# Second MoE's up products by seven block products instead of eight, with x2 kept in fp32

## What is computed

```
logits = x2 @ w_gate;  P = exp(logits - logits.max())
for _ in range(8):
    P /= P.sum(1, keepdims=True) + 1e-09
    P /= P.sum(0, keepdims=True) + 1e-09
    P *= N / E
for e in range(E):
    h = np.maximum(x2 @ w1[e], 0.0)
    out += P[:, e:e + 1] * (h @ w2[e])
```

## Time and profile before

| | |
|---|---|
| median of 3 runs | 1305.37 us (1305.13 to 1306.25) |
| the profiled execution | 1304.42 us, of which 1302.6 us are the span |
| mean granted TensorE clock | 1.00 of full speed |
| PE busy | 1265.2 us, 97% of the span, 8109 matmuls |
| DVE, ACT, POOL busy | 50%, 35%, 28% |

### The profile page before, as it was taken

How to read it: one execution, slowest core, us unless ns; L and a number is a source line. 1 busy time by engine, 2 the same in 40 slices (tenths; PEclk the granted TensorE clock), 3 DMA queues, 4 the chain that set the end, 5 groups by cost and what they waited for, 6 DMA issues and landing times.

```text
span 1302.6 us, 21366 instructions
## 1 busy us (share of the span) xinstructions
PE 1265.2 (97%) x8109; PEld 1119.5 (86%) x8109; DVE 653.2 (50%) x1557; ACT 458.6 (35%) x960; POOL 365.7 (28%) x319
## 2 busy tenths in 40 slices
PE   6999999999999999999999999999999999999999
PEld 5777787887887998899899899898898898998997
DVE  5999999999998237322222222222222222222222
ACT  4776666766766233022022032031131130220210
POOL 2774434524434223033032031131131130230300
PEclk9999999999999999999999999999999999999999
DMA  4875664654544643021021120020120220210001
GB/s 129 275 245 181 255 221 127 231 186 171 208 178 156 259 162 98 1 65 50 17 65 33 32 64 32 32 64 17 48 64 1 64 64 0 64 60 5 0 0 72
DMA packets 72929, 130.14 MB, mean 100 GB/s; under 512 B 42016, under 2 KB 42016, under 8 KB 63648
## 3 DMA queue, kind: packets, MB, share of 16 engines
q1 hardware_dynamic: 72864, 129.27, 29.3%
HBM read 110.12 MB, written 19.14 MB: 99 GB/s over the span
## 4 chain that ended last, share of the span: by engine, by line
PE 79%; DVE 16%; ACT 1%; SPq 1%; DMA 1%; issue 1%; POOL 1%; ACTq 0%; DVEq 0%
PE banks L409 25%; PE banks L411 24%; PE banks L410 24%; DVE stats L862 7%; DVE rest L873 6%; PE banks L477 2%; PE banks L444 1%; PE banks L453 1%; DVE g_f L927 1%; PE banks L470 1%; DMA q_nat<-in_q_dram 1%; SPq L333 1%; PE banks L500 0%; ACT pT L705 0%; PE banks L425 0%
## 5 line engine op out<-in xcount | busy, mean ns | idle before, releaser
L822 ACT ACTIVATE h_hi<-banks 128x384 fp32r<-128x384 f32 x192 | 94.4, 492 | 624.7 <-PE banks L411 624.7
L409 PE MATMUL banks<-x_lo,wu_hi 128*128 128x384 f32 x768 | 257.2, 335 | 0.0
L411 PE MATMUL banks<-x_hi,wu_hi 128*128 128x384 f32 x768 | 256.8, 334 | 0.0
L410 PE MATMUL banks<-x_hi,wu_lo 128*128 128x384 f32 x768 | 256.8, 334 | 0.0
L988 DVE SCALAR_TENSOR_TENSOR h_lo<-banks,h_hi 128x384 fp32r<-128x384 f32 x192 | 106.8, 557 | 281.7 <-ACT h_hi L822 281.7
L1087 POOL TENSOR_TENSOR wu_lo<-wu_raw,wu_hi 128x512 fp32r<-128x512 f32 x76 | 95.9, 1299 | 526.1 <-ACT wu_hi L761 519.1
L1030 DVE SCALAR_TENSOR_TENSOR y_acc<-banks,plan_e,y_acc 128x512 f32<-128x512 f32 x135 | 101.3, 751 | 272.3 <-PE banks L411 272.3
L409 PE MATMUL banks<-wd_lo,h_hi 128*128 128x512 f32 x576 | 227.9, 396 | 0.0
L411 PE MATMUL banks<-wd_hi,h_hi 128*128 128x512 f32 x576 | 227.8, 396 | 0.0
L410 PE MATMUL banks<-wd_hi,h_lo 128*128 128x512 f32 x576 | 227.8, 396 | 0.0
L862 DVE MAX8 stats<-rest 128x8 f32<-128x576 f32 x216 | 156.1, 750 | 0.7
(11 more groups left out here) (103 smaller groups left out, 1804.7 us busy)
## 6 DMA issues: line engine op xcount, KB each, us to landing
wu_raw<-in_moe_w_dram SPq DMA_DIRECT2D x32, 512.0 KB, 3.7
wd_raw<-in_moe_w_dram SPq DMA_DIRECT2D x32, 512.0 KB, 3.7
wu_hi<-kept_up_hi SPq DMA_DIRECT2D x14, 1024.0 KB, 5.6
wu_lo<-kept_up_lo SPq DMA_DIRECT2D x14, 1024.0 KB, 8.0
wd_hi<-kept_down_hi SPq DMA_DIRECT2D x14, 1024.0 KB, 6.3
wd_lo<-kept_down_lo SPq DMA_DIRECT2D x14, 1024.0 KB, 8.4
q_nat<-in_q_dram SPq DMA_DIRECT2D x64, 72.0 KB, 2.3
wu_raw<-in_moe_w_in_dram SPq DMA_DIRECT2D x8, 512.0 KB, 5.3
```

What stands on the lines that cost most here:

```text
L409: pe.matmul(to, a_hi, b_lo, start=first, stop=False)
L410: pe.matmul(to, a_lo, b_hi, start=False, stop=False)
L411: return pe.matmul(to, a_hi, b_hi, start=False, stop=last)
L822: act.activation(h_hi[:, f, CH * c:CH * (c + 1)], ps_up[:, at % UBANKS, 0:CH], ACT.Relu).then_inc(h_hi_done, 1)
```

## The change

- **Up products.** The 2x2 blocks are: D in two halves (256 each), hidden columns in two halves (256 of a unit's 512), tokens in two halves (576 each). Strassen's scheme in Winograd's form makes the four output blocks from 7 products of block sums instead of 8 products. A unit is 4 cells; a cell is one of 2 blocks of 128 hidden columns by one of 2 token quarters of each half (288 tokens). A cell has 7 products of 6 matmuls with 288 columns: 168 matmuls for each unit.
- **Outputs.** Products 0 to 3 fill four banks, 4, 5 and 6 are added by PE onto banks 0, 2 and 3. ACT copies product 0 out (P1); DVE forms U2, U3, H22, H21, H12 in SBUF with five additions; ACT makes four ReLUs and DVE four low parts of 288 columns.
- **Weights.** w1 is summed on POOL (4 operations of 128x512 for each unit), cast in 7 pieces on ACT and lowered in 7 pieces on POOL, into one buffer instead of two; the casts wait for the unit's last up product. w2 keeps two slots; its four casts stand on ACT after cell 2.
- **x2.** It stays fp32, so `sums_high`, `sums_low` and `split_sums` go. Its 7 operands for each of 2 token quarters are summed on DVE (4), cast on ACT (7) and lowered on DVE (7), 128x576 each: for c = 0 in steps 85 to 90, for c = 1 two at step 98 to 100, the rest after x2 is complete.
- **Logits.** 36 fp32 matmuls with x2 as weights and 8 columns moving, after x2 is complete, write the transposed logits straight away. The two chunks at step 88 go.
- **Down products.** Tiles go in the order 0, 1, 5, 2, 3, 4, 6, 7, 8; the first three need only cells 0 and 1. `y_acc` shares its memory with x2. Units 0 and 1 are added unscaled, and 9 `scale_tile` operations of DVE scale the sum after unit 1. The plan's rounds: two `column_sums` in unit 0's up part, three in its down part, three in unit 1's up part.

```diff
+PRODUCTS = 7
+BANK_OF = (0, 1, 2, 3, 0, 2, 3)
+CELLS = [(f, c) for c in range(2) for f in range(2)]
+DOWN_TILES = (0, 1, 5, 2, 3, 4, 6, 7, 8)
+EARLY_TILES = 3
...
 # PE
+            def logits_of(t):
                 for a in range(KD):
+                    last = pe.matmul(ps_gate[:, E * t:E * (t + 1)], x2[:, a, P * t:P * (t + 1)], gate_raw[:, a, :],
+                                     start=a == 0, stop=a == KD - 1)
...
+            def product(he, cell, i):
+                f, c = CELLS[cell]
+                k = len(CELLS) * he + cell
+                if i == 0:
+                    need(pe, h_lo_done, 4 * (k - 1) + 2)
+                elif i == 1:
+                    need(pe, summed, 5 * (k - 1) + 1)
+                elif i == 2:
+                    need(pe, summed, 5 * (k - 1) + 4)
+                elif i == 3:
+                    need(pe, summed, 5 * k)
+                elif i == 4:
+                    pe.wait_ge(p1_copied, k + 1)
+                else:
+                    pe.wait_ge(summed, 5 * k + i - 3)
+                if cell == 0:
+                    pe.wait_ge(lo_split["up"], up_lows(UQ + he) + i + 1)
+                for a in range(2):
+                    last = three_passes(ps_up[:, BANK_OF[i], 0:QT], w1_hi[:, i, a, cols], w1_lo[:, i, a, cols],
+                                        xo_hi[c][:, i, a, :], xo_lo[c][:, i, a, :], i < 4 and a == 0, a == 1, i >= 4)
...
 # ACT
+            for place in range(2, PRODUCTS):
+                x_high(1, place)
+            act.wait_ge(xo_lo_done, 2 * PRODUCTS)
...
+            def cell_high(he, cell):
+                need(act, summed, 5 * (k - 1) + 1)
+                act.wait_ge(up2_done, PRODUCTS * k + 1)
+                act.copy(parts_f32[:, P1, :], ps_up[:, 0, 0:QT]).then_inc(p1_copied, 1)
+                act.wait_ge(summed, 5 * k + 3)
+                relu(2 + f, tokens_of(1, c), parts_f32[:, H22, :])
+                act.wait_ge(up2_done, PRODUCTS * k + 5)
+                relu(f, tokens_of(0, c), ps_up[:, 0, 0:QT])
+                act.wait_ge(summed, 5 * k + 4)
+                relu(2 + f, tokens_of(0, c), parts_f32[:, H21, :])
+                act.wait_ge(summed, 5 * k + 5)
+                relu(f, tokens_of(1, c), parts_f32[:, H12, :])
             def expert(he, slot, first, last):
+                for cell in range(len(CELLS)):
+                    cell_high(he, cell)
+                    if cell == 2 and not last:
...
+                        w2_high(he + 1, 1 - slot)
+                if not last:
+                    act.wait_ge(up2_done, PRODUCTS * len(CELLS) * (he + 1))
+                    for i in range(PRODUCTS):
+                        w1_high(he + 1, i)
...
 # DVE
+            def cell_sums(he, cell):
...
+                add(part[U2], bank[1], part[P1])
+                add(part[U3], bank[2], part[U2])
+                add(part[H22], bank[3], part[U3])
+                low(2 + f, tokens_of(1, c), part[H22])
+                low(f, tokens_of(0, c), bank[0])
+                add(part[H21], bank[2], part[U2])
+                add(part[H12], bank[3], part[U2])
+                low(2 + f, tokens_of(0, c), part[H21])
+                low(f, tokens_of(1, c), part[H12])
...
+            def scale_tile(at):
+                t = DOWN_TILES[at]
+                dve.wait_ge(y_added, TT + at + 1)
+                dve.tensor_scalar(y_acc[:, t, :], y_acc[:, t, :], plan[:, t, 0:1], None,
+                                  ALU.mult).then_inc(y_added, 1)
...
 # POOL
             with pool.Fori(1, E) as e:
                 for half in range(HALVES):
-                    split("up", UQ + HALVES * e + half, half)
-                    split("down", UQ + HALVES * e + half, half)
+                    w2_lows(HALVES * e + half, half)
+                    w1_sums(HALVES * e + half)
+                    w1_lows(HALVES * e + half)
```

More of the change, by code:

```diff
@@ L47 @@
 NU2 = E * HALVES
-CH = 384
-NCH = N // CH
 TT = N // P
 SLOTS = 2
-UBANKS, DBANKS = 4, 3
-ROUND_AFTER = [(3, 3), (5, 1), (6, 3), (8, 1), (9, 3), (11, 1)]
+DBANKS = 3
+PRODUCTS = 7
+BANK_OF = (0, 1, 2, 3, 0, 2, 3)
+HF = UNIT // 2
+CELLS = [(f, c) for c in range(2) for f in range(2)]
+DOWN_TILES = (0, 1, 5, 2, 3, 4, 6, 7, 8)
+EARLY_TILES = 3
+U2, U3, H22, H21, H12, P1 = range(6)
+X_ORDER = (0, 4, 6, 3, 1, 2, 5)
+X_SUMS = (3, 1, 2, 5)
 LOWEST = -3.4028234663852886e38
@@ L342, in load_half, with load_expert @@
                 sp.dma_start(raw[stream][:, parts, :], source[:, parts, :]).then_inc(loaded[stream][half], 16)
-            def load_unit(stream, n, source):
-                for half in range(2):
-                    load_half(stream, n, source, half)
+            def load_expert(he, e, half):
+                sp.wait_ge(lo_split["up"], up_lows(UQ + he))
+                for part in range(2):
+                    parts = slice(part * PARTS // 2, (part + 1) * PARTS // 2)
+                    sp.dma_start(wu_raw[:, parts, :], w1_u[e, half][:, parts, :]).then_inc(loaded["up"][part], 16)
+                for part in range(2):
+                    load_half("down", UQ + he, w2_u[e, half], part)
             def load_split(stream, n, half):
@@ new lines, in _ @@
+                if step == ALL + 6:
+                    x_high(0, 2)
+                    x_high(0, 3)
+                if step == ALL + 7:
+                    x_high(0, 4)
+                    x_high(0, 5)
+                if step == ALL + 9:
+                    x_high(0, 6)
+                if step == ALL + 18:
+                    act.wait_ge(up_done, UF * NU1)
+                    for i in range(PRODUCTS - 1):
+                        w1_high(0, i)
+                if step == ALL + 19:
+                    act.wait_ge(g_lo_done, UF * NU1)
+                    x_high(1, 0)
+                    x_high(1, 1)
@@ L825, in expert @@
             def expert(he, slot, first, last):
-                for at in range(UF * NCH):
-                    if first and at == 1:
+                for cell in range(len(CELLS)):
+                    cell_high(he, cell)
+                    if first and cell == 1:
                         act.wait_ge(all_max, 2)
@@ L1045, in _ @@
             dve.wait_ge(plan_exp, 1)
-            taken = 1
-            for round_ in range(SINK):
-                rows(round_)
-                after = ROUND_AFTER[round_] if round_ < len(ROUND_AFTER) else (UF * NCH, 0)
-                while taken <= after[0] - (after[1] < KD - 1):
-                    h_low(0, taken)
-                    taken += 1
-                columns(round_)
-            expert_column(0)
-            for t in range(TT):
-                add_tile(0, t)
-            expert(1)
+            rows(0)
@@ new lines, in _ @@
+            cell_sums(0, 2)
+            columns(0)
+            rows(1)
+            cell_sums(0, 3)
+            columns(1)
+            rows(2)
+            for at in range(TT):
+                add_tile(0, at)
+                if at % 3 == 2:
+                    columns(2 + at // 3)
+                    rows(3 + at // 3)
+            for cell in range(3):
+                cell_sums(1, cell)
+                columns(5 + cell)
+                if cell < 2:
+                    rows(6 + cell)
@@ L1059, in _ @@
+            cell_sums(1, 3)
+            for at in range(TT):
+                add_tile(1, at)
+            for at in range(TT):
+                scale_tile(at)
             with dve.Fori(1, E) as e:
```

444 lines of the change are left out of this document (251 added, 193 removed).

## The result

The changed kernel takes **1289.46 us** in the median of 4 runs (1287.47 to 1292.18); the kernel before, on the same chip, 1305.78 (1305.13 to 1306.25). The ratio is 0.9875, 95% interval 0.9863 to 0.9887: faster by 16 us, where 27 were forecast. That is inside the forecast range of 1268 to 1291, 1.5 us from its upper edge. The profiled execution took 1287.5 us with a span of 1285.7; that of before is 1302.6, so the traces differ by 16.9 us.

The account below looks back on a forecast made before the run. PE's matmuls were taken as the bound. Terms -35.8 + 7.0 - 4.2 + 2.4 + 1.0 + 1.3 + 0.7 + 1.0 - 0.5 = -27.1 took 1304.4 to 1277.3, forecast 1278 us; range 1268 to 1291, its own 1272 to 1285.

Parts of the forecast that it names:

- the clock's rival: Unit 0's logits: PE's clock falls on 8-column matmuls, +4 us there and +4 in products after; 1286 us, chance 0.13.
- Part 1: Up matmuls, units 1 to 15: 168 at 134.4 ns, 22.6 us a unit against 24.98; -35.8 us if PE never waits.
- Part 2: ACT and DVE work in each cell: a cell by itself costs PE nothing, with margins of 0.4 to 1.8 us.
- That rival: Cells wait at more places: 0.3 us lost in each of 60 cells, +18, 1296 us; chance 0.12.
- Part 3: Four w2 casts on ACT before cell 3's P1 copy: 0.5 us in each of units 1 to 14, +7.0 us.
- Part 4: POOL's weight work, 18.8 us a unit instead of 10: costs nothing, hidden behind down matmuls with 10.8 us to spare.
- Part 5: Logits and unit 0: removed chunks -4.2 us; last feed-forward slice to end of unit 0's up part, 35.1 against 32.7, +2.4.
- the term of 9.0 us for the logits: Unit 0's logits: 36 fp32 matmuls of two instructions, 0.25 us a pair, 9.0 us; bounds 5 and 18.
- The weighed rule on SBUF: DVE operations with two SBUF inputs and POOL block each other; low parts after cell 3 have 8 us slack, so nothing added.
- Part 6: Small terms: column sums +1.0, scale_tile +1.3, rounds in unit 1 +0.7, x2 sums +1.0, removed sums and gate split -0.5.
- The three terms up to the last slice: Before unit 0: removed logits chunks -4.2 us, x2 sums for c = 0 +1.0, removed sums and gate split -0.5.
- The signs named ahead: Down parts 25.2 us, about 14 P1 waits of 0.3; wrong if cells wait, up parts exceed 24 or the clock dips.

Follow-up runs that it names:

- the kernel with six early tiles: Changed kernel with w2 casts after cell 3, scaling after each addition, and six tiles' logits between slices of the last feed-forward quarter: 1271.54 us, ratio 0.9732.
- the repeat: Changed kernel with w2 casts after cell 3, scaling between additions and logits with 128 columns moving, run again in 5 rounds: 1270.11 us, ratio 0.9711.

## Why the prediction was right, and where it was off

Right were the direction, what bounds the kernel, and the wide range; the gain was 10 us smaller than the sum. The forecast's own range, 1272 to 1285, was missed, and the wide one held 1289.46 because it took in the clock's rival and part of another. Step by step:

- **Part 1 held.** 133.2 ns for a matmul instead of 134.4, 22.38 us instead of 22.6. The product 15 x 2.4 is 36.0, not 35.8 (from 22.6 it would be 35.7); without waits 38.9 is measured, 3.1 us better.
- **Part 2 held.** With the casts out of the way no cell waits (22.38 us), so the margins of 0.4 to 1.8 us are real. That rival is refuted.
- **Part 3 named the right place and order but was mis-sized, the largest error in the units.** ACT began the casts 6.63 us into cell 2 and ended them at 8.71 (6.64 and 8.72 forecast), product 4 was 0.34 us late (0.3). What was short is the step behind: "U3 then ends at 10.1 [...] 0.1 more". DVE began its sums 0.22 us after ACT's end, as it did at 13 such sums, not the 0.04 of the earlier trace rows. Those sums have three waits, that for ACT first of the three; in the kernel with six early tiles the first one had nothing else to wait for and began 0.03 us behind ACT. So the waits behind the first are the likely cause, though nothing was tried on it. Product 5 started 0.37 us late on top, 0.1 of it product 4's restart, and its own restart cost 0.1 more. Measured 0.66 in unit 1, 0.83 in unit 2, 1.20 in unit 3 and about 0.84 or 0.95 by turns behind it, 12.4 in all instead of 7.0: **5.4 us**.
- **Part 4 held.** POOL's last low part of w1 ends at 739.75, unit 5 begins at 749.90: 10.1 us to spare (10.8 forecast). Its four low parts took 5.03 us.
- **Part 5: the rival with the clock came in.** The pace taken, 0.25 us for a pair, was itself pessimistic (0.22 at full clock), so with the fall (5.0 us in the logits, where the rival had 4) the stretch up to the first product was 13.8 us instead of 10.0. Another 1.4 us went in the products behind it (the rival had 4). The rival's 1286 us is near what was measured, but only because the casts, which it left at 7.0, made up the rest. The step that failed is the term of 9.0 us for the logits, which held full clock throughout, and the 0.13 given to the fall. It took the nearest rows for the thing itself: the instructions of the earlier trace rows have 128 columns moving, and the clock rose while they ran; with 8 columns it fell. Cells and column sums of unit 0 took 27.2 us instead of 25.1.
- **The weighed rule on SBUF.** "The sum has nothing for it" was wrong for unit 0: POOL's first low parts come in cell 1 or 2, and the second four end just where cell 3's sums are due. L1153 stretched from 0.17 to 0.89, L1155 from 0.23 to 1.00, two low parts from 0.83 to 2.95, while the reduction and the reciprocal between them, with one input each, stayed at 0.23 and 0.21. The Trainium skill's rule (SBUF — State Buffer, "Who interferes with whom") agrees; what it needed was a look at which round meets which POOL operation. In steady units the prediction was right: two DVE low parts at 726.57 were held to 3.07 us and nobody waited.
- **Part 6.** `scale_tile` measured 2.4 us against 1.3: nine operations took 3.65 us instead of 3.1, the wait of 2.03 was paid in full, and the restart came on top. The rounds in unit 1's cells with their three column sums took 1.84 us (24.22 instead of 22.38 without the casts) against 0.7 and 0.75: 0.4 more. The three terms up to the last slice (-4.2, +1.0, -0.5) measured -3.5 together.

- **The signs named ahead.** Down parts took 25.2 us, and PE stood behind ACT's P1 copy 13 times, 0.2 us each (14 and 0.3 forecast). Against them: 6.3 us of waits for DVE's sums where hardly any were forecast, up parts over 24 us in units 0 to 2 (27.2, 24.9 and 25.7), and a dip in the clock row. The last two had been named as signs of being wrong, and they point at Part 5 and Part 6.

Together: -3.1 + 5.4 + 1.1 + 0.4 in units 1 to 15, +5.9 from the last slice to the end of unit 0's up part, +0.2 ahead of it: 9.9 of the 10.2 us by which the profiled run missed the sum.

## What to carry to other kernels

When a change makes the bound engine's work shorter, walk one period of the others against it, with hand-over times from rows that have as many waits as the new code, and count a restart (0.1 us here) for each late group: half the gain hung on where four casts stood. Small operations of a vector engine that share SBUF with POOL's are to be placed by when POOL works, and a faster stretch ahead moves them onto it. Rows of matmuls with few columns deserve a look at the granted clock; making them wider can be cheaper than making them fewer.

## What the runs showed of the hardware

- PE is shown busy without a gap, and the clock falls: 8 columns moving, 0.11 us an instruction, half clock from 488.1 on for 13.7 us in the changed kernel, for 17 in four others, for 10 in two. 128 columns at the same 0.11 us held 1.00 through the logits and the first products in three profiles. The Trainium skill (TensorE: Matmul & The Clock Gate, "What's actually happening") speaks of activity that releases the throttle; here the throttle came back while PE was shown busy.
- An fp32 instruction with new weights took 0.11 us at full clock with 8 columns moving and with 128, and 0.21 at half clock with 8.
- Short falls of about 3.4 us came with some idle spells of PE, not all: with one of 1.88 us (casts in two pairs), with 2.57 and 2.93 us (early tiles), with 3.22 us (the repeat), with 2.04 us near 81 us in the changed kernel's profile (at the same place that of before shows none); and none with 2.27 us in unit 0 of the changed kernel or 3.04 us with wide logits alone. So the length of the spell alone does not decide, and what does is open. It is part of the spread between runs of one kernel: the repeat took 1265.78 us at a mean clock of 1.000 and 1270.46 at 0.996.
- A `partition_all_reduce` on POOL prints 0.38 us (0.64 at most), and POOL's next operation began some 7 us after it in every trace ("7.46 <-issue"); this fixes when the first low parts of w2 run. What POOL does there wasn't tried.
